# A couple's split moved to the end of its own step, and its inverse twiddle product moved behind the output product

## The chip, the cores and the metric

One NeuronCore of one Trainium2 chip runs the whole kernel. The metric is the device time of one execution in microseconds; the time before is the median of three runs. The profile and the trace are of one more execution.

## The reference, cut to what matters

```
X  = rfft(x, axis=1)                    # x: 4 x 3008 x 256
Yr = Xr @ w_r - Xi @ w_i + b_r
Yi = Xr @ w_i + Xi @ w_r + b_i
Yr, Yi = sign(Y) * max(|Y| - 0.01, 0)   # each part by itself
y  = irfft(Yr + 1j * Yi, n=3008)
h  = y @ w_in                           # 12032 x 256 times 256 x 2048
out = (max(h, 0) + alpha * min(h, 0)) @ w_out
```

## The kernel before

**Numbers.** Every product is made from float32 operands that are split into a rounded part `hi` and a rest `lo`; a product is then three matmuls, hi*hi, hi*lo and lo*hi. A split is a copy on ACT (ScalarE) that makes `hi`, followed by a subtraction on DVE (VectorE) or POOL (GpSimd) that makes `lo`.

**The transforms.** The 3008 points are 94 x 32. A forward transform has a product over 94 points (`forward1`), a trip through DRAM, and a product with twiddle factors (`forward2`), which gives one *unit* of 128 spectrum rows. There are 24 units for each of the four batch rows. Units are handled two at a time as a *couple*: `mix_couple` multiplies both with the mixing weights, `bias_couple` adds the bias, `above_couple` and `shrink_couple` threshold, `split_couple` (ACT, L734) and `rest_couple` (DVE, L963) split the thresholded result `shrunk` into `shr_hi` and `shr_lo`. `inverse2` (PE, L536), once for each unit of the couple, multiplies them with the inverse twiddle factors into PSUM bank 2 of `work_ps`. `copy_couple` (ACT, L739) copies both results to `inv_sb`, and `store_couple` (SP, L330) stores them to DRAM. From there `load_back`, `split_back` and `inverse1` (PE, over 94 points) bring the activations `y`.

**The feed-forward loop.** The main loop has 24 tiles `f` of 502 or 500 tokens, each with 16 steps `m`. In a step PE does `hidden(f, m)` (six matmuls into one of the two banks of `h_ps`), then whatever the transforms have in this step, then `output` of the step two before (LAG = 2; six matmuls into `out_ps`). ACT makes `negpart` of the hidden product (`bend`, L785) and then `g_hi` of the step before (`split_bent`, L794). DVE makes `g_raw` (`bend`, L1008) and then `g_lo` of the step before (`rest_bent`, through the helper at L911). `hidden` waits until the bank it writes has been read by DVE's `bend` two steps earlier; `output(q)` waits for `g_lo` of its step, which DVE makes in its step q + 1, behind `bend(q + 1)`.

**Order.** Each engine works through a list of its own, written out by hand, and stops at a wait until the semaphore is there. For a batch row 1, 2 or 3 the units are spread over a period of 96 steps. Unit j of 24 stands at step 22 + (9 * j // 4) of the period, and odd j closes a couple. With T for that step, the couple's work stands, through `p_couple(f, m, after)` (L78), at these steps before the change:

| step | work of the couple |
| --- | --- |
| T + 2 | `mix_couple` (PE), `bias_couple` (DVE) |
| T + 3 | `above_couple` (ACT), `shrink_couple` (DVE), `split_couple` (ACT, last of the step) |
| T + 4 | `rest_couple` (DVE) |
| T + 5 | `inverse2` twice (PE, ahead of `inverse1` and `output`), `copy_couple` (ACT, in the middle of the step) |
| T + 6 | `store_couple` (SP) |

The next couple's T is 4 or 5 steps later, in turn. Where it is 4, the steps T + 2 and T + 4 hold a unit and T + 3 and T + 5 hold none; where it is 5, the steps T + 3 and T + 5 hold a unit. A unit's step has, on PE, `forward2`; on ACT, `copy_more`, `split_whole`, `split_sum` and for every third unit `split_itw`, a split of the table; on DVE, `whole_spec` and `rest_whole`; on POOL, `sum_spec` and `rest_sum`. Two steps before a unit stand `split_pair` (ACT) and `rest_pair` (DVE). `inverse1` and its splits (`i_unit`, L89) stand at even steps m from 4 on, four to six of them for a tile; `split_back` (ACT) at m = 2, 6 and 10; the transposes of the finished tile (`turn`, DVE) at m = 1.

```
p = p_couple(f, m, 5)
if p is not None:
    inverse2(p - 1)
    inverse2(p)
```

The buffers `shrunk`, `shr_hi`, `shr_lo` and `above` hold one couple. `split_couple` waits for the couple's `shrunk` and for the couple before to have passed `inverse2`. The last third of `mix_couple` writes PSUM bank 2 and waits for `copy_couple` of the couple before.

Of the kernel before, what the change touches and what calls it, by code (L numbers as in the profile page):

```python
# [68 lines left out]
def p_unit(f, m, after):  # L69

    at = f % 6 * STEPS + m - after - 22
    for j in range(PAIRS):
        if f < TILES - 6 and at == 9 * j // 4:
            return PAIRS * (f // 6 + 1) + j
    return None


def p_couple(f, m, after):  # L78

    p = p_unit(f, m, after)  # L80
    return p if p is not None and p % 2 else None
# [19 lines left out]
def mixer_kernel(nc, x, w_r, w_i, b_r, b_i, w_in, w_out, alpha, dft, idft, twiddles, out):  # L101
    with ExitStack() as ctx:  # L102
# [355 lines left out]
        def _(pe):  # L458
# [77 lines left out]
            def inverse2(p):  # L536
                t, k = p // 3 % 2, p % 3
                if k == 0:
                    pe.wait_ge(itw_lo_done, p // 3 + 1)
                pe.wait_ge(shr_lo_done, p + 1)  # L540
                if 2 <= p < PAIRS:
                    pe.wait_ge(inv_copied, p - 1)
                hi, lo = shr_hi[:, p % 2, :], shr_lo[:, p % 2, :]
                product(inv_bank(p), [(itw_hi[:, t, k, :], hi), (itw_hi[:, t, k, :], lo), (itw_lo[:, t, k, :], hi)]
                        ).then_inc(inv_mm, 1)
# [45 lines left out]
            def output(f, m):  # L591
                q = f * STEPS + m
                size = TILE_AT[f % 3][1]
                pe.wait_ge(g_lo_done, q + 1)
                if q == 0:
                    pe.wait_ge(y_lo_done, I_HEAD)
                if f == 0 and m % 2 == 0:
                    pe.wait_ge(wout_lo_done, m // 2 + 1)
                gh, gl = g_hi[:, q % 3, 0:size], g_lo[:, q % 3, 0:size]
                for h in range(DH):  # L600
                    if m == 0 and f >= 1:
                        pe.wait_ge(turned_done, 2 * f - 1 + h)
                    d = slice(h * P, (h + 1) * P)
                    hi, lo = wout_hi[:, m // 2, m % 2, d], wout_lo[:, m // 2, m % 2, d]
                    mm = product(out_ps[:, h, 0:size], [(hi, gh), (hi, gl), (lo, gh)], first=m == 0, last=m == STEPS - 1)
                    if h == 0 and m == STEPS - 1:
                        mm.then_inc(out_half, 1)
                mm.then_inc(out_mm, 1)
# [33 lines left out]
            for f in range(TILES):  # L642
                for m in range(STEPS):
                    hidden(f, m)
                    s = s_unit(f, m)
                    if s is not None:
                        forward1(s)
                    p = p_couple(f, m, 2)
                    if p is not None:
                        mix_couple(p)  # L650
                    p = p_unit(f, m, 0)
                    if p is not None:
                        forward2(p)
                    p = p_couple(f, m, 5)
                    if p is not None:
                        inverse2(p - 1)
                        inverse2(p)
                    u = i_unit(f, m)
                    if u is not None:
                        inverse1(u)  # L660
                    q = f * STEPS + m - LAG
                    if q >= 0:
                        output(*divmod(q, STEPS))
            for m in range(STEPS - LAG, STEPS):
                output(TILES - 1, m)

        @block.scalar
        def _(act):
# [65 lines left out]
            def split_couple(p):  # L734
                act.wait_ge(shrunk_done, p + 1)
                act.wait_ge(inv_mm, p - 1)
                act.activation(shr_hi[:, :, :], shrunk[:, :, :], ACT.Copy).then_inc(shr_hi_done, 2)  # L737

            def copy_couple(p):  # L739
                act.wait_ge(inv_mm, p + 1)  # L740
                if p == PAIRS + 1:
                    for k in range(2):
                        act.wait_ge(inv_stored[k], 16 * GROUPS)
                else:
                    act.wait_ge(couple_stored, 16 * (p - PAIRS - 1) // 2)
                act.activation(inv_sb[:, 0:2, :], work_ps[:, 2, :].rearrange("p (q d) -> p q d", q=2),
                               ACT.Copy).then_inc(inv_copied, 2)
# [25 lines left out]
            def split_y(u):  # L773
                act.wait_ge(back_mm, u + 1)
                if y_free(u) > 0:
                    act.wait_ge(h_mm, STEPS * y_free(u))
                act.activation(y_place(y_hi, u), i_views(u)[0], ACT.Copy).then_inc(y_hi_done, 1)
# [81 lines left out]
            for f in range(TILES):  # L859
                for m in range(STEPS):  # L860
                    bend(f, m)
                    q = f * STEPS + m
                    if q >= 1:
                        split_bent(*divmod(q - 1, STEPS))
                    s = s_unit(f, m)
                    if s is not None:
                        copy_fwd(s)
                    if f == 1 and m in (1, 2):
                        split_mixw(m)
                    p = p_couple(f, m, 3)  # L870
                    if p is not None:
                        above_couple(p)
                    p = p_unit(f, m, 0)
                    if p is not None:
                        copy_more(p)
                    p = p_couple(f, m, 5)
                    if p is not None:
                        copy_couple(p)
                    u = i_unit(f, m)
                    if u is not None:  # L880
                        split_y(u)
                    p = p_unit(f, m, 0)
                    if p is not None:
                        split_whole(p)
                    p = p_unit(f, m, -2)
                    if p is not None:
                        split_pair(p)
                    v = i_bpair(f, m - 2)
                    if v is not None:
                        split_back(v)  # L890
                    if f == 0 and m % 2 == 0 and m // 2 + 2 < CHUNKS:
                        split_ffw(m // 2 + 2)
                    p = p_unit(f, m, -2)
                    if p is not None and p % 3 == 0:
                        split_tw(p // 3)
                    p = p_unit(f, m, 0)
                    if p is not None:
                        split_sum(p)
                        if p % 3 == 0:
                            split_itw(p // 3)  # L900
                    p = p_couple(f, m, 3)
                    if p is not None:
                        split_couple(p)
            split_bent(TILES - 1, STEPS - 1)
            for n in range(1, 12, 2):
                store_out(act, TILES - 1, n)
# [2 lines left out]
        def _(dve):  # L909
# [192 lines left out]
            for f in range(TILES):  # L1102
                for m in range(STEPS):
                    bend(f, m)
                    q = f * STEPS + m
                    if q >= 1:
                        rest_bent(*divmod(q - 1, STEPS))
                    if f >= 1 and m == LAG - 1:
                        turn(f - 1, 0)
                        turn(f - 1, 1)  # L1110
                    if s_unit(f, m + 2) is not None:
                        split_x(s_unit(f, m + 2), False)
                    p = p_couple(f, m, 4)
                    if p is not None:
                        rest_couple(p)
                    p = p_couple(f, m, 3)
                    if p is not None:
                        shrink_couple(p)
                    p = p_couple(f, m, 2)
                    if p is not None:  # L1120
                        bias_couple(p)
                    p = p_unit(f, m, 0)
                    if p is not None:
                        whole_spec(p)
                    u = i_unit(f, m)
                    if u is not None:
                        rest_y(u)
                    p = p_unit(f, m, 0)
                    if p is not None:
                        rest_whole(p)  # L1130
                    if f == 0 and m % 2 == 0 and m // 2 + 2 < CHUNKS:
                        rest_win(m // 2 + 2)
                    p = p_unit(f, m, -2)
                    if p is not None:
                        rest_pair(p)
# [162 lines left out]
```

## Time and profile before

| quantity | value |
| --- | --- |
| median of three runs | 1444.81 us (1444.39 to 1447.1) |
| the profiled execution | 1444.94 us |
| its span, first to last instruction | 1443.1 us |
| mean granted clock of TensorE | 0.991 of full speed |
| busy share: PE, DVE, ACT, POOL | 97%, 65%, 52%, 21% |

The span leaves out 1.8 us of the profiled execution's time, around the first and the last instruction. PE is TensorE; a busy PE is one with a matmul in flight, and since the ends of matmuls are modelled and overlap, a loss of PE time is read from the starts of its matmuls.

### The profile page before, as it was taken

To read this page: it belongs to the slowest core of one execution; us is meant where nothing else is said; L and a number is where in the kernel's file an instruction comes from. 1 tells how busy PE (TensorE), PEld (TensorE's weight loads), DVE (VectorE), ACT (ScalarE), POOL (GpSimd) and SP (SyncE) were. 2 spreads that over 40 slices of the span, in tenths; PEclk is the share of its full clock that TensorE was granted. 3 is DMA by queue.
4 is the path that set the end of the run, shared out by engine and by line. 5 is a ranking of instruction groups with operands and counts; after the bars stand their busy time and mean duration, and the time that the engine had idled before them with its cause. 6 is when DMAs were issued, how large, how long until landed. Compare 5 with 4: busy or idle time off the path is not lost. (4 is left out here: it accounts for less than half of the span.)

```text
span 1443.1 us, 21507 instructions
## 1 busy us (share of the span) xinstructions
PE 1393.5 (97%) x7012; PEld 1171.1 (81%) x7012; DVE 942.3 (65%) x1824; ACT 743.9 (52%) x1646; POOL 301.7 (21%) x351
## 2 busy tenths in 40 slices
PE   8998999999999999998999999999999999999997
PEld 4987888878888888887888888887888888888886
DVE  5786777777765557777775656776776555555554
ACT  3775555555544545655554445565555444444433
POOL 0433532222201422222210241221220110001000
PEclk9999999999999999999999999999999999999999
DMA  6654522122210541213211242222120111001100
GB/s 216 188 153 129 151 66 72 51 63 59 53 38 15 134 107 52 66 47 77 56 33 38 59 114 74 57 67 61 51 55 21 31 26 27 17 19 31 21 15 14
DMA packets 163114, 94.68 MB, mean 66 GB/s; under 512 B 110500, under 2 KB 140628, under 8 KB 163004
## 3 DMA queue, kind: packets, MB, share of 16 engines
q1 hardware_dynamic: 158250, 88.91, 23.4%
q10 hardware_dynamic: 4754, 4.41, 1.0%
q8 instruction: 56, 0.92, 0.3%
q14 instruction: 54, 0.44, 0.1%
HBM read 55.74 MB, written 37.49 MB: 65 GB/s over the span
## 5 line engine op out<-in xcount | busy, mean ns | idle before, releaser
L1008 DVE SCALAR_TENSOR_TENSOR g_raw<-negpart,keep,h_ps 128x502 f32<-128x502 f32 (+1 forms) x384 | 282.8, 736 | 412.9 <-ACT negpart L785 408.0
L785 ACT ACTIVATE negpart<-h_ps 128x502 f32<-128x502 f32 (+1 forms) x384 | 224.7, 585 | 488.8 <-PE h_ps L461 488.8
L461 PE MATMUL out_ps<-g_hi,wout_hi 128*128 128x502 f32 (+1 forms) x768 | 311.9, 406 | 2.8 <-DVE g_lo L911 1.3
L461 PE MATMUL h_ps<-y_hi,win_hi 128*128 128x502 f32 (+1 forms) x768 | 301.2, 392 | 0.6 <-DVE g_raw L1008 0.3
L461 PE MATMUL h_ps<-y_lo,win_hi 128*128 128x502 f32 (+1 forms) x768 | 300.9, 392 | 0.0
L461 PE MATMUL out_ps<-g_hi,wout_lo 128*128 128x502 f32 (+1 forms) x768 | 300.6, 391 | 0.0
L461 PE MATMUL h_ps<-y_hi,win_lo 128*128 128x502 f32 (+1 forms) x768 | 299.9, 390 | 0.0
L461 PE MATMUL out_ps<-g_lo,wout_hi 128*128 128x502 f32 (+1 forms) x768 | 299.8, 390 | 0.0
L911 DVE TENSOR_TENSOR g_lo<-g_raw,g_hi 128x502 fp32r<-128x502 f32 (+1 forms) x384 | 267.9, 698 | 0.1
L794 ACT ACTIVATE g_hi<-g_raw 128x502 fp32r<-128x502 f32 (+1 forms) x384 | 235.9, 614 | 0.3 <-DVE g_raw L1008 0.3
L461 PEld LDWEIGHTS h_ps<-y_hi,win_hi 128*128 128x128 f32 x768 | 146.1, 190 | 32.1 <-DVE y_lo L911 0.8
L461 PEld LDWEIGHTS out_ps<-g_hi,wout_hi 128*128 128x128 f32 x768 | 145.6, 190 | 31.5 <-issue 6.2
L461 PEld LDWEIGHTS h_ps<-y_hi,win_lo 128*128 128x128 f32 x768 | 144.9, 189 | 30.7
L461 PEld LDWEIGHTS out_ps<-g_hi,wout_lo 128*128 128x128 f32 x768 | 145.5, 189 | 30.0
L461 PEld LDWEIGHTS h_ps<-y_lo,win_hi 128*128 128x128 f32 x768 | 145.6, 190 | 29.7
L1143 POOL TENSOR_TENSOR back_lo<-back_raw,back_hi 96x512 fp32r<-96x512 f32 x61 | 83.1, 1362 | 406.1 <-ACT back_hi L771 405.9
L461 PEld LDWEIGHTS out_ps<-g_lo,wout_hi 128*128 128x128 f32 x768 | 146.2, 190 | 22.0
L1165 POOL TENSOR_TENSOR room<-room 128x128 f32<-128x128 f32 x72 | 33.1, 459 | 395.0 <-DVE room L933 395.0
L1143 POOL TENSOR_TENSOR x_lo<-x_raw,x_hi 94x512 fp32r<-94x512 f32 x44 | 56.7, 1289 | 103.7 <-DVE x_hi L917 103.7
L718 ACT ACTIVATE spec_hi<-room 128x256 fp32r<-128x256 f32 x72 | 30.1, 418 | 90.9 <-DVE room L933 90.9
L461 PE MATMUL work_ps<-mixw_lo,spec_hi 128*128 128x256 f32 x216 | 61.0, 282 | 0.0
L461 PE MATMUL work_ps<-mixw_hi,spec_hi 128*128 128x256 f32 x216 | 60.9, 282 | 0.0
(117 smaller groups left out, 1976.4 us busy)
## 6 DMA issues: line engine op xcount, KB each, us to landing
pair_raw<-fwd_scratch SPq DMA_DIRECT2D x96, 128.0 KB, 2.1
back_raw<-inv_scratch SPq DMA_DIRECT2D x61, 192.0 KB, 2.5
table<-in_twiddles_dram SPq DMA_DIRECT2D x28, 384.0 KB, 3.4
x_raw<-in_x_dram SPq DMA_DIRECT2D x64, 160.0 KB
inv_scratch<-inv_sb SPq DMA_DIRECT2D x36, 256.0 KB, 2.2
fwd_scratch<-staging SPq DMA_DIRECT2D x44, 192.0 KB, 2.1
out_dram<-turned SPq DMA_DIRECT2D x124, 40.0 KB, 2.0
inv_scratch<-inv_sb SPq DMA_DIRECT2D x24, 128.0 KB, 2.8
```

Source lines behind the costliest of these rows:

```text
L461: mm = pe.matmul(ps, lhs, rhs, start=(first and n == 0), stop=(last and n == len(terms) - 1), **kw)
L718: act.activation(three(spec_hi)[:, :, 0:2, p % 2, :], spec, ACT.Copy).then_inc(spec_hi_done, 1)
L785: act.activation(negpart[:, q % 2, 0:size], h_ps[:, q % 2, 0:size], ACT.Relu, scale=-1.0).then_inc(negpart_done, 1)
L794: act.activation(g_hi[:, q % 3, 0:size], g_raw[:, q % 2, 0:size], ACT.Copy).then_inc(g_hi_done, 1)
L911: return dve.tensor_tensor(dst, whole, hi.bitcast(F32), ALU.subtract)
L1008: dve.scalar_tensor_tensor(g_raw[:, q % 2, 0:size], negpart[:, q % 2, 0:size], keep[:, m:m + 1], h_ps[:, q % 2, 0:size], ALU.mult, ALU.add ...
L1143: return pool.tensor_tensor(dst, whole, hi.bitcast(F32), ALU.subtract)
L1165: pool.tensor_tensor(spec_sum, spec[:, :, 0, :], spec[:, :, 1, :], ALU.add).then_inc(sum_done, 1)
```

## The change

`rest_couple` moves from DVE's step T + 4, where it stood ahead of `shrink_couple`'s place, to the step T + 3, behind `rest_whole` and ahead of `rest_pair`. `split_couple` moves within ACT's step T + 3 from the last place to the place behind `split_y` and ahead of `split_whole`, `split_pair` and `split_back`. The two `inverse2` stay in step T + 5 and move on PE from the place ahead of `inverse1` to the place behind `output`. `copy_couple` stays in ACT's step T + 5 and moves from the middle of the step to its last place. `store_couple` stays where it is. No instruction is added or taken away, and no wait is changed.

```diff
--- before.py
+++ after.py
@@ -651,16 +651,16 @@
                     p = p_unit(f, m, 0)
                     if p is not None:
                         forward2(p)
-                    p = p_couple(f, m, 5)
-                    if p is not None:
-                        inverse2(p - 1)
-                        inverse2(p)
                     u = i_unit(f, m)
                     if u is not None:
                         inverse1(u)
                     q = f * STEPS + m - LAG
                     if q >= 0:
                         output(*divmod(q, STEPS))
+                    p = p_couple(f, m, 5)
+                    if p is not None:
+                        inverse2(p - 1)
+                        inverse2(p)
             for m in range(STEPS - LAG, STEPS):
                 output(TILES - 1, m)
 
@@ -873,12 +873,12 @@
                     p = p_unit(f, m, 0)
                     if p is not None:
                         copy_more(p)
-                    p = p_couple(f, m, 5)
-                    if p is not None:
-                        copy_couple(p)
                     u = i_unit(f, m)
                     if u is not None:
                         split_y(u)
+                    p = p_couple(f, m, 3)
+                    if p is not None:
+                        split_couple(p)
                     p = p_unit(f, m, 0)
                     if p is not None:
                         split_whole(p)
@@ -898,9 +898,9 @@
                         split_sum(p)
                         if p % 3 == 0:
                             split_itw(p // 3)
-                    p = p_couple(f, m, 3)
-                    if p is not None:
-                        split_couple(p)
+                    p = p_couple(f, m, 5)
+                    if p is not None:
+                        copy_couple(p)
             split_bent(TILES - 1, STEPS - 1)
             for n in range(1, 12, 2):
                 store_out(act, TILES - 1, n)
@@ -1110,9 +1110,6 @@
                         turn(f - 1, 1)
                     if s_unit(f, m + 2) is not None:
                         split_x(s_unit(f, m + 2), False)
-                    p = p_couple(f, m, 4)
-                    if p is not None:
-                        rest_couple(p)
                     p = p_couple(f, m, 3)
                     if p is not None:
                         shrink_couple(p)
@@ -1128,6 +1125,9 @@
                     p = p_unit(f, m, 0)
                     if p is not None:
                         rest_whole(p)
+                    p = p_couple(f, m, 3)
+                    if p is not None:
+                        rest_couple(p)
                     if f == 0 and m % 2 == 0 and m // 2 + 2 < CHUNKS:
                         rest_win(m // 2 + 2)
                     p = p_unit(f, m, -2)
```

## Rows read from the trace of the kernel before

**Rows 1.** The page: busy us of each engine, share of the span, instructions.

```profile
PE 1393.5 (97%) x7012; PEld 1171.1 (81%) x7012; DVE 942.3 (65%) x1824; ACT 743.9 (52%) x1646; POOL 301.7 (21%) x351
```

**Rows 2.** Waits of PE from 200 us on: total us, times, longest us.

```profile
PE work_ps L461 <- DVE shr_lo L911: 25.1, 30, 3.4
```

**Rows 3.** The same view for one period, 205 to 416 us.

```profile
PE work_ps L461 <- DVE shr_lo L911: 8.4, 10, 3.4
```

**Rows 4.** Timeline, first couple: start us, us, engine, operation [idle before <-releaser].

```profile
216.07 0.63 ACT L737 ACTIVATE shr_hi<-shrunk 128x512 fp32r<-128x512 f32 x1 [1.14 <-issue]
...
216.61 0.57 ACT L785 ACTIVATE negpart<-h_ps 128x502 f32<-128x502 f32 x1
...
217.87 0.68 DVE L911 TENSOR_TENSOR g_lo<-g_raw,g_hi 128x502 fp32r<-128x502 f32 x1
...
217.97 0.39 PE L461 MATMUL h_ps<-y_lo,win_hi 128*128 128x502 f32 x1
...
218.21 0.38 PE L461 MATMUL h_ps<-y_hi,win_lo 128*128 128x502 f32 x1
...
218.46 0.68 DVE L911 TENSOR_TENSOR shr_lo<-shrunk,shr_hi 128x512 fp32r<-128x512 f32 x1
...
219.29 0.36 PE L461 MATMUL work_ps<-shr_hi,itw_hi 128*128 128x256 f32 x1 [0.70 <-DVE shr_lo L911]
```

**Rows 5.** Timeline, second couple, whose steps also hold units.

```profile
229.75 0.69 DVE L960 SCALAR_TENSOR_TENSOR shrunk<-biased,above 128x512 f32<-128x512 f32 x1
...
230.81 0.42 ACT L718 ACTIVATE spec_hi<-room 128x256 fp32r<-128x256 f32 x1 [0.94 <-DVE room L933]
...
231.64 0.62 ACT L737 ACTIVATE shr_hi<-shrunk 128x512 fp32r<-128x512 f32 x1
...
233.41 0.67 DVE L911 TENSOR_TENSOR g_lo<-g_raw,g_hi 128x502 fp32r<-128x502 f32 x1
...
233.96 0.22 PE L496 MATMUL work_ps<-tw_parts,pair_lo 128*128 128x128 f32 x1
...
234.74 0.39 PE L461 MATMUL work_ps<-shr_hi,itw_hi 128*128 128x256 f32 x1 [0.56 <-DVE shr_lo L911]
```

**Rows 6.** Timeline, third couple, with an inverse1 product in the same step.

```profile
251.92 0.67 DVE L911 TENSOR_TENSOR g_lo<-g_raw,g_hi 128x500 fp32r<-128x500 f32 x1
...
252.45 0.38 PE L461 MATMUL h_ps<-y_hi,win_lo 128*128 128x500 f32 x1
...
254.06 0.25 PE L567 MATMUL work_ps<-idft_parts,back_hi 96*128 96x188 f32 x1
...
254.44 0.46 PE L461 MATMUL out_ps<-g_hi,wout_hi 128*128 128x500 f32 x1
```

**Rows 7.** Timeline, sixth couple, the longest wait of the period.

```profile
302.43 0.61 ACT L737 ACTIVATE shr_hi<-shrunk 128x512 fp32r<-128x512 f32 x1
...
304.21 0.68 DVE L911 TENSOR_TENSOR g_lo<-g_raw,g_hi 128x502 fp32r<-128x502 f32 x1
...
304.62 1.38 POOL L1143 TENSOR_TENSOR back_lo<-back_raw,back_hi 96x512 fp32r<-96x512 f32 x1 [0.95 <-ACT back_hi L771]
...
304.80 1.76 DVE L911 TENSOR_TENSOR shr_lo<-shrunk,shr_hi 128x512 fp32r<-128x512 f32 x1
...
306.61 0.39 PE L461 MATMUL work_ps<-shr_hi,itw_hi 128*128 128x256 f32 x1 [3.37 <-DVE shr_lo L911]
```

**Rows 8.** Durations of one kind: ns min/median/max, first and last start.

```profile
L911 DVE TENSOR_TENSOR shr_lo<-shrunk,shr_hi x60: 424/682/1759, 43.8 to 1104.2; 128x512 fp32r<-128x512 f32 x36, 128x256 fp32r<-128x256 f32 x24
...
L771 ACT ACTIVATE back_hi<-back_raw x62: 615/622/637, 111.6 to 1362.7; 96x512 fp32r<-96x512 f32 x62
```

**Rows 9.** Busy us by stretches; last three columns: granted clock, DMA share, GB/s.

```profile
307.53:310.94 3.41, 3.41 (x10) 2.72 (x9) 1.36 (x4) 1.41 (x4) 0.99 (x2) 0.50 0.51 150
...
652.28:655.69 3.41, 3.18 (x11) 2.83 (x12) 2.26 (x6) 1.40 (x4) 0.46 (x1) 0.50 0.15 30
...
997.02:1003.85 6.83, 5.50 (x16) 4.73 (x17) 3.61 (x6) 1.92 (x6) 1.71 (x3) 0.50 0.50 136
```

## The prediction, made before the changed kernel ran

> **What bounds the kernel now.** I read four views, in this order. First the page: PE is busy for 97% of the span, DVE for 65% [rows 1]. So only what makes PE stand still, or run slowly, is worth anything. Second, the waits of PE in the main loop, where one line holds nearly all: the inverse twiddle products (on `work_ps`) wait for DVE's `shr_lo`, 25.1 us in 30 waits [rows 2]. Third, the same view for one period of 96 steps: 8.4 us in 10 waits, the longest 3.4 [rows 3]; the other two periods repeat it to the digit. Twelve couples stand in a period, so two of them do not wait. Fourth, the timeline around single waits, to see what is late and why.
>
> A wait's listed idle time is not the whole loss. Matmuls of `hidden` start 0.23 us apart (217.97 to 218.21, with rounding), so after the one at 218.21 the next could start at 218.44; it starts at 219.29. That is 0.85 lost where the row lists 0.70 [rows 4]. With 0.16 more for each wait a period loses 8.4 + 10 x 0.16 = 10.0 us, and the three periods 30.0 us. In period order, the ten losses are 0.85, 0.72, 0.58, 0.80, 3.54 (sixth couple), 0.85, 0.79, 0.57, 0.78 and 0.48 (they are the ten idle times plus 0.16; they add up to the 10.0; rows 4 to 7 show the first, second, third and sixth couple).
>
> In the first couple one sees the mechanism. ACT ends `shr_hi` at 216.70. DVE could subtract then, but its list has `bend` and `rest_bent` of step T + 4 first, so `shr_lo` starts at 218.46 only, behind `g_lo`, and ends at 219.14. PE stands from 218.44 on [rows 4].
>
> Beside the waits there are three stretches in which the granted clock is 0.50, the 1.2 GHz level: 3.41, 3.41 and 6.83 us [rows 9]. Each begins about when a 3.4 us idle stretch of PE ends, that of the sixth couple of a period [rows 7]. They sum to 13.65 us; at half rate they cost at most 6.8 us.
>
> **The change part by part.** Nothing is added: the same instructions run. The sum is only of waits removed and waits that appear.
>
> *rest_couple into T + 3.* One DVE operation, 0.68 us [rows 8], 36 times in the loop. `shr_lo` is then ready about two steps before `inverse2` needs it, so all 30.0 us of the waits for it go. What is late next: `output` of step T + 3, which in T + 5 now comes ahead of `inverse2` and needs `g_lo` of its step. DVE makes that behind `bend` of T + 4, and ahead of that now stands `shr_lo`.
>
> Couples without a unit in T + 3 and T + 5. In the first, `shr_lo` would run from 216.78 to 217.46, overlapping `negpart` (216.61 to 217.18) [rows 4]. `bend` starts at 217.40 where it could start at 217.21, 0.19 later; `g_lo` ends at 218.55 + 0.19 = 218.74; with 0.1 to reach PE, `output` starts at 218.84. PE is there at 218.44, so 0.40 is lost in place of 0.85. The old product started 0.74 behind the end of `g_lo`, the new one 0.29 behind its old end: each such loss shrinks by 0.45. For 0.57 and 0.48 that leaves 0.12 and 0.03. Where `inverse1` is in T + 5, it now runs before `output` and gives the others 0.38 more (254.06 to 254.44 [rows 6]): of 0.58 nothing is left.
>
> Couples with a unit in T + 3. *split_couple ahead of split_whole*: ACT stood idle for 0.94 before `split_whole`, waiting for DVE; `shrunk` is done at 230.44, `split_whole` starts at 230.81, `shr_hi` at 231.64 [rows 5]. `shr_hi` would run from 230.50 to 231.12, `split_whole` 0.23 later than before, and all behind it ends 0.3 earlier. On DVE `rest_whole` waits 0.23 longer, then `shr_lo` and `rest_pair` follow, and `bend` of T + 4 starts about where it did; `g_lo` ends at 234.08 + 0.05. `output` starts at 234.23; PE is there at 234.74 - 0.72 = 234.02. Each such loss shrinks by 0.51: 0.72 to 0.21, 0.80 with an `inverse1` to 0, and 0.78 to between 0 and 0.27; I take 0.2.
>
> Two couples have a `split_back` in T + 3, a copy of 0.62 us [rows 8], that ran while ACT waited for `shrunk` or `rest_whole`, and now runs behind `split_couple`. In the one without a unit (0.85, `inverse1` present) it pushes `negpart` by up to 0.62; the loss is 0.85 - 0.45 - 0.38 + 0.6, less the 0.19 that `shr_lo` no longer pushes: 0.4. In the other (0.79) POOL's subtraction of that load may now start before DVE's `rest_pair`, which is bounded below; I take 0.4 there too.
>
> The sixth couple. `shr_hi` starts at 302.43, behind four other operations of ACT; `g_lo` is done at 304.89; then `shr_lo` takes 1.76 us [rows 7], where the median is 0.68 [rows 8]. It started 0.18 behind a subtraction of POOL that lasts 1.38. In its new place, about 302.2, it starts before POOL's load work and should take 0.7. The chain through ACT shrinks by 0.3, `g_lo` ends at 304.6, `output` starts at 304.7 and PE is there at 306.61 - 3.54 = 303.07: 1.6 lost in place of 3.54.
>
> The couples that did not wait stay at nothing. A period then loses 0.40 + 0.21 + 0 + 0 + 1.6 + 0.4 + 0.4 + 0.12 + 0.2 + 0.03 = 3.4 us in place of 10.0. Three periods save 3 x 6.6 = 19.8 us.
>
> *A meeting with POOL* bounds this from the other side. A DVE subtraction that starts under one of POOL's is longer by up to 1.76 - 0.68 = 1.08 us. If every moved `shr_lo` met one, 36 x 1.08 = 39 us would be added to DVE's list, at most that to PE. If none does, nothing is added. I am near the lower end, since one in twelve does now. On this the Trainium skill ("SBUF — State Buffer", section "Who interferes with whom") says that a DVE instruction with two SBUF inputs and a GpSimd instruction that reads SBUF exclude each other, and that the second to start blocks entirely until the first ends. By that the operation of 304.80 would end 1.20 + 0.68 = 1.88 later; the row has 1.76, so it bears the rule out but for 0.12. It speaks against this change, because every place of `shr_lo` that falls behind a POOL start is charged with POOL's rest; it is rival 3 below.
>
> *inverse2 behind output, copy_couple last.* Six matmuls keep their length. Behind `inverse2` on PE stands only the next `hidden`, which needs nothing from it. `copy_couple` waits at the end of ACT's step T + 5, and behind it stands `negpart` of T + 6, which cannot start before `hidden` of T + 6 ends, 1.4 us after `inverse2`; the copy is shorter. The last third of `mix_couple`, where it comes in T + 6, starts another 1.4 us later. In SP's list `store_couple` may hold `load_pair` and `load_back` by 1 to 2 us; these run several steps ahead. So zero for this part; without that cover it could cost its lateness, up to about 1 us a couple or 36 us, but neither loads nor `inv_sb` show up in PE's waits now. A gain from the order alone is in the 0.38 above.
>
> *The clock.* A PE idle stretch of 1.6 us in place of 3.5 may or may not be followed by the lower level; stretches of 0.9 and less in the loop are not. Between 0 and 6.8 us come back. I take half, 3.4.
>
> Sum: 19.8 + 3.4 = 23.2. The profiled execution took 1444.94 us (span 1443.1 and 1.8 around it), 0.1 above the median of the runs: 1444.9 - 23.2 = 1421.7, so 1422.
>
> **The rivals.** (1) *Everything goes*: the new waits for `g_lo` are hidden too, and the clock never drops. 30.0 + 6.8 gone gives 1408. For it: DVE has 35% to spare. Against it: ACT's chain in the sixth couple is 2 us late by itself. (2) *The wait changes its name*: `shr_lo` delays `g_lo` by its full 0.68, not by 0.19 or 0.05. The new losses are then about 0.5 to 0.6 larger in each of the ten, less where `inverse1` covers: 3.4 + 4.2 = 7.6 a period, saving 3 x 2.4 = 7 us, 1437 to 1438. For it: both stand on the same list. Against: `bend` has to wait for `negpart` anyway, with DVE idle. (3) *Slower, by POOL*: the moved `shr_lo`, or `rest_pair` behind it, starts under a POOL subtraction and stretches to 1.76 in nearly all couples, so that `g_lo` is 1.08 + 0.19 late. A period would lose 3.4 + 12 x 1.08, less 1.5 of slack: 14.9 in place of 10.0, and the time is 1444.9 + 3 x 4.9 = 1460. It decides from 6.6 / 12 = 0.55 us of added lateness per couple; above that the change is slower. Against: POOL is busy for 21% of the span, and DVE's earlier start should mostly come first. (4) *No effect*: ACT makes `shr_hi` so late in either order that `shr_lo` is not earlier: 1444.9. Rows 4 speak against it: `shr_hi` ended 1.76 us before `shr_lo` began.
>
> **How the numbers follow.** Forecast (1415 to 1431) 0.70, rival 1 0.10, rival 2 0.11, rival 3 0.04, rival 4 0.05. The likeliest case gives 1422. The range takes most of the forecast's own and the near parts of rivals 1 and 2: 1411 to 1435. What a measurement of this kernel can tell from no change is 0.2%, 2.9 us. Faster: forecast, rivals 1 and 2, 0.91. Same: rival 4, and a mild form of rival 3, 0.05. Slower: 0.04.
>
> **What would show it.** In the profile after, PE's waits for `shr_lo` in the loop should be near 0 in place of 25.1; waits of `out_ps` for `g_lo` should appear, about 20 of them with 8 to 10 us of loss in total, the longest near 1.5 three times. DVE's `shr_lo` of 512 columns should have 0.68 as its maximum, not 1.76. The stretches at half clock should be fewer or gone. PE's idle time before `inverse2` should be 0. It would be wrong if `g_lo`'s waits total above 20 us (rival 2), if `shr_lo`, `pair_lo` or `g_lo` have a mean well above 0.7 (rival 3), or if a wait of `work_ps` for `inv_sb` or of `negpart` behind `copy_couple` shows that the copy was not free.

## The result, and the profile after

The changed kernel takes 1421.31 us, median of four runs (1420.35 to 1423.1), where the kernel before, run beside it, takes 1445.95 us. The ratio is 0.983, interval 0.9812 to 0.9848: 24.6 us faster. The forecast was 1422, of a range of 1411 to 1435. The profiled execution took 1423.1 us with a span of 1421.3.

The waits of PE from 200 us on, kernel after (total us, times, longest us), answer to [rows 2]:

```profile
PE out_ps L461 <- DVE g_lo L911: 4.2, 10, 0.7
PE work_ps L495 <- DVE pair_lo L911: 2.1, 3, 0.7
PE out_ps L461 <- DVE turned L1057: 0.8, 5, 0.2
```

The 25.1 us for `shr_lo` are gone. Two smaller waits stand in their place: `output` for `g_lo`, which was expected, and `forward2` for `pair_lo`, which was not. One of the ten waits for `g_lo`, of 0.7, stands at the end of the loop, as it did before the change.

The first couple, kernel after, answers to [rows 4]:

```profile
218.21 0.63 ACT L737 ACTIVATE shr_hi<-shrunk 128x512 fp32r<-128x512 f32 x1 [1.15 <-issue]
218.95 0.69 DVE L911 TENSOR_TENSOR shr_lo<-shrunk,shr_hi 128x512 fp32r<-128x512 f32 x1 [0.82 <-ACT shr_hi L737]
219.56 0.73 DVE L1008 SCALAR_TENSOR_TENSOR g_raw<-negpart,keep,h_ps 128x502 f32<-128x502 f32 x1
220.21 0.67 DVE L911 TENSOR_TENSOR g_lo<-g_raw,g_hi 128x502 fp32r<-128x502 f32 x1
220.35 0.38 PE L461 MATMUL h_ps<-y_hi,win_lo 128*128 128x502 f32 x1
220.94 0.49 PE L461 MATMUL out_ps<-g_hi,wout_hi 128*128 128x502 f32 x1 [0.20 <-DVE g_lo L911]
222.40 0.28 PE L461 MATMUL work_ps<-shr_hi,itw_hi 128*128 128x256 f32 x1
```

`shr_lo` now comes before `bend` and `g_lo`. PE could have started at 220.58 and starts `output` at 220.94, when `g_lo` is there: 0.35 lost where 0.85 was, and `inverse2` follows with no wait.

The sixth couple, kernel after, answers to [rows 7]:

```profile
302.28 0.69 DVE L911 TENSOR_TENSOR shr_lo<-shrunk,shr_hi 128x512 fp32r<-128x512 f32 x1
302.49 0.79 POOL L1143 TENSOR_TENSOR spec_lo<-room,spec_hi 128x128 fp32r<-128x128 f32 x1 [0.73 <-ACT spec_hi L722]
302.88 0.68 DVE L911 TENSOR_TENSOR pair_lo<-pair_raw,pair_hi 128x256 fp32r<-128x256 f32 x1
303.24 1.19 POOL L1143 TENSOR_TENSOR itw_lo<-table,itw_hi 128x384 fp32r<-128x384 f32 x1
303.61 0.38 PE L495 MATMUL work_ps<-tw_parts,pair_hi 128*128 128x256 f32 x1 [0.71 <-DVE pair_lo L911]
304.13 0.83 DVE L911 TENSOR_TENSOR g_lo<-g_raw,g_hi 128x502 fp32r<-128x502 f32 x1
305.02 0.50 PE L461 MATMUL out_ps<-g_hi,wout_hi 128*128 128x502 f32 x1 [0.74 <-DVE g_lo L911]
```

Here are two losses, 0.88 at `forward2` (0.71 listed and 0.17 more) and 0.90 at `output`; together 1.78 in place of 3.54. DVE and POOL are seen in turn behind each other: `pair_lo`, now behind `shr_lo`, starts under POOL's operation and takes 0.68, where its median is 0.42.

**The balance.** The losses of one period, from the starts of the matmuls as in the prediction:

| couple | 1 | 2 | 3 | 4 | 5 | 6 | 7 | 8 | 9 | 10 | 11 | 12 | sum |
| --- | --- | --- | --- | --- | --- | --- | --- | --- | --- | --- | --- | --- | --- |
| before | 0.85 | 0.72 | 0.58 | 0.80 | 0 | 3.54 | 0.85 | 0.79 | 0.57 | 0.78 | 0.14 | 0.48 | 10.1 |
| forecast | 0.40 | 0.21 | 0 | 0 | 0 | 1.6 | 0.4 | 0.4 | 0.12 | 0.2 | 0 | 0.03 | 3.4 |
| after | 0.35 | 0.40 | 0 | 0.17 | 0 | 1.78 | 0.27 | 0.30 | 0.16 | 0.13 | 0 | 0 | 3.6 |

(The 0.14 of the eleventh couple has no idle time listed, since it is shorter than the modelled tail of the matmul before; the prediction missed it.) Three periods save 30.3 - 10.7 = 19.6 us. In the loop the three half-clock stretches of [rows 9] are gone, and most of the rest is theirs. The loop, seen from the first and last start of `g_raw` (ns min/median/max, first and last start us; first the kernel before, then after), shows it:

```profile
L1008 DVE SCALAR_TENSOR_TENSOR g_raw<-negpart,keep,h_ps x384: 717/737/743, 124.2 to 1431.9; 128x502 f32<-128x502 f32 x128, 128x500 f32<-128x500 f32 x64
```

```profile
L1008 DVE SCALAR_TENSOR_TENSOR g_raw<-negpart,keep,h_ps x384: 718/737/742, 125.8 to 1410.1; 128x502 f32<-128x502 f32 x128, 128x500 f32<-128x500 f32 x64
```

The loop went from 1307.7 to 1284.3 us, 23.4 less: 19.6 of waits and 3.8 of everything else. The clock alone gave more than 3.8. Two of PE's matmuls in the first half-clock stretch of the kernel before start 0.42 apart, where the same two are 0.23 apart at the full clock:

```profile
308.57 0.62 PE L461 MATMUL out_ps<-g_hi,wout_hi 128*128 128x502 f32 x1
308.99 0.62 PE L461 MATMUL out_ps<-g_lo,wout_hi 128*128 128x502 f32 x1
```

Added up over all starts, the three stretches cost 1.5, 1.5 and 2.6 us, 5.6 in all. Two smaller things go the other way in the kernel after: about 1.1 us in delays of under 0.11 each, most of them at the second matmul behind a wait, which no row of the table counts, and 0.6 us in the loop's first 27 steps, where the clock was still at 0.50 until 127.16. 19.6 + 5.6 - 1.1 - 0.6 is the 23.4 but for 0.1. Ahead of the loop 1.6 us were lost in this execution, where the clock was at 0.50 for longer (kernel after, then before; the last three columns are granted clock, DMA share and GB/s):

```profile
110.10:127.16 17.06, 16.55 (x57) 13.92 (x56) 5.61 (x12) 5.85 (x13) 0.29 (x1) 0.50 0.33 109
```

```profile
44.70:48.12 3.42, 3.42 (x18) 3.42 (x18) 2.02 (x5) 1.78 (x5) 1.53 (x2) 0.50 0.69 193
116.38:123.21 6.83, 6.58 (x23) 5.50 (x23) 1.50 (x5) 1.20 (x4) 0.00 (x0) 0.50 0.56 182
```

The change touches nothing there. 23.4 - 1.6 is the difference of the spans, 21.8.

### The profile page after: what moved, and what is told of

Its sections match the earlier page's. It is cut to its first block and busy times, and to the rows that moved or that the text cites. A ratio compares the mean times of both kernels' runs of the same rounds, so it can differ in the third digit from the quotient of the medians.

```text
span 1421.3 us, 21507 instructions
## 1 busy us (share of the span) xinstructions
PE 1391.1 (98%) x7012; PEld 1168.1 (82%) x7012; DVE 949.9 (67%) x1824; ACT 744.2 (52%) x1646; POOL 306.7 (22%) x351
## 5 line engine op out<-in xcount | busy, mean ns | idle before, releaser
L911 DVE TENSOR_TENSOR g_lo<-g_raw,g_hi 128x502 fp32r<-128x502 f32 (+1 forms) x384 | 271.0, 706 | 0.1
L461 PE MATMUL work_ps<-mixw_hi,spec_lo 128*128 128x256 f32 x216 | 60.8, 282 | 0.0
```

Of the source, the lines that this page charges most:

```text
L461: mm = pe.matmul(ps, lhs, rhs, start=(first and n == 0), stop=(last and n == len(terms) - 1), **kw)
L911: return dve.tensor_tensor(dst, whole, hi.bitcast(F32), ALU.subtract)
```

## The experiments

Each was run in rounds beside the kernel before. `[D]`, `[A]`, `[P]` and `[C]` name the four moves of the change: `rest_couple` on DVE, `split_couple` on ACT, `inverse2` on PE, `copy_couple` on ACT.

| kernel | moves | median us | ratio to before, interval | loss per period |
| --- | --- | --- | --- | --- |
| the full change | D A P C | 1421.31 | 0.9830 (0.9812 to 0.9848) | 3.6 |
| e1 | D | 1425.83 | 0.9866 (0.9851 to 0.9880) | 4.7 |
| e2 | D A | 1413.76 | 0.9788 (0.9775 to 0.9802) | 1.7 |
| e3 | P C | 1421.69 | 0.9835 (0.9815 to 0.9854) | 2.7 |
| e4 | D A, `rest_pair` first | 1413.35 | 0.9785 (0.9772 to 0.9799) | 1.7 |
| e5 | D A P | 1421.22 | 0.9830 (0.9815 to 0.9845) | 3.6 |
| e6 | A P C | 1417.18 | 0.9797 (0.9782 to 0.9813) | 2.3 |
| e7 | D A P C, `rest_pair` first | 1419.92 | 0.9819 (0.9804 to 0.9833) | 3.2 |
| e8 | A | 1445.88 | 0.9999 (0.9986 to 1.0012) | 9.8 |
| e9 | e4, sixth couple as before | 1425.25 | 0.9855 (0.9837 to 0.9873) | 4.2 |
| e10 | before, sixth couple as e4 | 1433.80 | 0.9911 (0.9895 to 0.9927) | 7.5 |
| e11 | e4, `rest_tw` first | 1411.05 | 0.9749 (0.9733 to 0.9766) | 1.1 |

e9, e10 and e11 ran in other rounds than e1 to e8. There the kernel before took 1446.68 us, beside the others 1444.93 to 1445.95, so a distance of 1 to 2 us between medians of different rounds says little.

### The split without the product's move: e1 and e2

e1 moves `rest_couple` alone. e2 adds `split_couple`:

```diff
+p = p_couple(f, m, 3)      # e2: ACT, ahead of split_whole; e1: left last in the step
+if p is not None:
+    split_couple(p)
+p = p_couple(f, m, 3)      # both: DVE, behind rest_whole
+if p is not None:
+    rest_couple(p)
```

> Only rest_couple moves (DVE, step T + 4 to T + 3); ACT's and PE's lists are those of the kernel before. Theory A (PE's loss came from shr_lo standing behind bend and rest_bent, and each product behind it covers what the next operand is late): the waits for shr_lo vanish, but DVE now stands at shr_hi, which ACT still makes last in T + 3, with rest_pair behind it. The sixth couple keeps about 2.7 us of loss, the four couples with a unit 0.2 to 0.7 each, at forward2 for pair_lo. Loss per period 4.3 us in place of 10.0: 17 us less, and 2 to 6 from the clock, about 1424. Rival B (the order on PE is what brings the gain: a product ahead of inverse2 covers its wait): this edit brings under 6 us, above 1439. Rival C (most of the gain is the clock level that no longer drops): as much as the full change only if the half-clock stretches go.

e1 measured 1425.83, where theory A said about 1424. The waits moved to `forward2`, as theory A had it, and in the sixth couple to `output` as well. Rival B falls: the move on DVE alone brings 19 us, with PE's list untouched. Rival C asked for the half-clock stretches. One of the three is gone and two are left, in the first and the third period, 3.41 us each; they cost 3.1 us by the starts of the matmuls. The first stands behind these two waits of the sixth couple:

```profile
302.18 0.39 PE L495 MATMUL work_ps<-tw_parts,pair_hi 128*128 128x256 f32 x1 [1.71 <-DVE pair_lo L911]
304.14 0.50 PE L461 MATMUL out_ps<-g_hi,wout_hi 128*128 128x502 f32 x1 [0.53 <-DVE g_lo L911]
```

```profile
304.52:307.93 3.41, 3.41 (x10) 2.72 (x9) 2.13 (x5) 0.92 (x3) 0.99 (x2) 0.50 0.82 245
```

The second period has the same two waits and no half-clock stretch.

> rest_couple and split_couple move as in the change; inverse2 and copy_couple stay where the kernel before has them. Theory A: inverse2 finds shr_lo ready and, standing ahead of output, gives g_lo 0.77 us more time. The waits of output for g_lo (0.35, 0.40, 0.90, 0.30, 0.16 in a period of the changed kernel) go but for 0.1; what is left is forward2's wait for pair_lo (0.88, 0.17, 0.13, 0.27). Loss per period 1.3 us in place of 3.6: 6 to 7 us faster than the changed kernel, about 1415. Rival B: slower than the changed kernel by several us, since its PE order is undone. Rival C: equal to the changed kernel, 1421.

e2 measured 1413.76, 7.5 us below the full change (theory A: 6 to 7). In its first couple, `inverse2` keeps PE busy while `g_lo` is made:

```profile
219.80 0.68 DVE L911 TENSOR_TENSOR g_lo<-g_raw,g_hi 128x502 fp32r<-128x502 f32 x1
219.94 0.39 PE L461 MATMUL h_ps<-y_hi,win_lo 128*128 128x502 f32 x1
220.17 0.28 PE L461 MATMUL work_ps<-shr_hi,itw_hi 128*128 128x256 f32 x1
...
220.88 0.39 PE L461 MATMUL out_ps<-g_hi,wout_hi 128*128 128x502 f32 x1
```

Its matmuls follow at 0.23 behind `hidden`, and `output` starts at 220.88 without a wait: the 0.35 of the changed kernel is 0. The product's move is what costs (e5 below shows that the copy's is free). Of the 7.5 us the table's losses give 3 x 1.9 = 5.7; the other 1.8 are fewer of the small delays at the second matmul behind a wait. Two losses of size are left in a period: 0.88 in the sixth couple, and 0.53 in the tenth, where `forward2` waits for POOL's `tw_parts` (1.1 us in 3 waits), which the expectation did not name.

### The product's move without the split's: e3, e6, e8

e3 leaves the split alone and moves `inverse2` and `copy_couple`. e6 adds `split_couple`. e8 moves `split_couple` alone. All three keep

```diff
 p = p_couple(f, m, 4)      # DVE, ahead of shrink_couple
 if p is not None:
     rest_couple(p)
```

> Only inverse2 moves behind output and copy_couple to the end of ACT's step; the split of the couple (split_couple, rest_couple) stays as before. Theory A: g_lo is made ahead of shr_lo as before, output starts when g_lo is there, and the output product (1.4 us) covers shr_lo. The losses per period are 0.2 for the first couple, 0.15 for the second, 1.9 to 2.2 for the sixth, 0 to 0.1 for the rest: 2.6 us, about as good as the full change: 1418 to 1421. If the wait only changed its name, the output product would now lose what inverse2 lost, and the time would stay above 1435. Rival B: all of the gain is here, 1421 or less, and e1 and e2 bring little. Rival C: the sixth couple's idle stretch is about 2 us in place of 3.4; if the clock still drops there, 2 to 5 us of the gain are missing.

e3's sixth couple (timeline):

```profile
301.34 0.68 DVE L911 TENSOR_TENSOR g_lo<-g_raw,g_hi 128x502 fp32r<-128x502 f32 x1
...
301.94 1.78 DVE L911 TENSOR_TENSOR shr_lo<-shrunk,shr_hi 128x512 fp32r<-128x512 f32 x1
302.07 0.49 PE L461 MATMUL out_ps<-g_hi,wout_hi 128*128 128x502 f32 x1 [1.69 <-DVE g_lo L911]
...
303.77 0.39 PE L461 MATMUL work_ps<-shr_hi,itw_hi 128*128 128x256 f32 x1
```

`output` covers nearly all of the 1.78 us that `shr_lo` takes. So either move by itself removes most of the loss, and the gains do not add. e3's loss of 2.7 is smaller than the full change's 3.6, yet its median is the same. Its profiled execution took 1416.69 at a mean granted clock of 0.996; the other three took 1420.52 to 1422.99 at 0.992 to 0.988. That is in line with a clock that drops behind the 1.69 us stretch in some executions. In the traced one it dropped behind none of the three; in e1's it did behind two of three waits of 1.7 us. The three slower executions of e3 had no trace, so for them it is not shown.

> The full change less the move of rest_couple: split_couple, inverse2 and copy_couple move, shr_lo is still made in T + 4 behind g_lo. Theory A: output waits for g_lo alone. Per period 0.16 for the first couple, 0.4 for the seventh (split_back behind split_couple), 1.6 for the sixth, 0.2 elsewhere: 2.4 us in place of 10.0, so 23 us less than the kernel before without the clock: 1417 if the clock never drops in the loop, 1420 to 1422 if the 1.6 us stretches still let it drop, as the spread of e3_pe_copy (1416.7 to 1423.0, mean granted clock 0.996 to 0.988) suggests. Rival (rest_couple's move is needed once inverse2 is late): above 1424.

e6 measured 1417.18, as if the clock never dropped, and its four runs had 0.994 to 0.996. It is the full change without `rest_couple`'s move, and it is 4 us faster. That is the plainest sign that, once `inverse2` stands behind `output`, making `shr_lo` early only delays `g_lo` and `pair_lo`.

> Only split_couple moves ahead of split_whole. Theory A: shr_lo stays behind bend and rest_bent of T + 4, so the losses stay; in the five couples with a unit ACT's chain is 0.28 shorter and each loses 0.3 less, the seventh couple loses 0.6 more, since split_back now runs ahead of negpart: 9.2 us a period in place of 10.0, 2 to 3 us less: 1442 to 1443. Rival (ACT's order is the cause of the late shr_lo): 1435 or less.

e8 measured no difference, where theory A said 1442 to 1443. The sixth couple lost 3.13, the second 0.44 and the seventh 1.45, as expected in place and sign, but the other couples with a unit gained 0.1 at most and not 0.3 (measured 0.71, 0.79 and 0.70 at the fourth, eighth and tenth). The rival fell, and theory A's sum for this kernel was 0.6 us a period too good.

### The side moves: e5, e7

e5 keeps the full change but for `copy_couple`; e7 puts `rest_couple` behind `rest_pair`:

```diff
+p = p_couple(f, m, 5)      # e5: ACT, ahead of i_unit, and not last in the step
+if p is not None:
+    copy_couple(p)
...
 p = p_unit(f, m, -2)       # e7: DVE
 if p is not None:
     rest_pair(p)
+p = p_couple(f, m, 3)      # and not behind rest_whole
+if p is not None:
+    rest_couple(p)
```

> The full change, but copy_couple stays in the middle of ACT's step T + 5, where it now waits for an inverse2 that comes only behind output. Theory A: ACT stands about 1 us at that wait and reaches split_y, split_whole and negpart of T + 6 1 to 1.5 us later; but mix_couple and the next output products give PE more than that, so PE loses 0 to 0.5 us a couple at most: 1421 to 1425, the same as the full change within 2 us if the cover holds. Rival: the move of copy_couple is what makes the late inverse2 affordable; then y_lo, spec_lo or g_lo are late in each of the 36 couples by about 0.5 us or more and the time is 1435 or above.

1421.22: the same waits to the digit (`g_lo` 4.2 us in 10, `pair_lo` 2.1 in 3). Moving the copy was worth nothing and cost nothing; the cover held.

> The full change with rest_couple behind rest_pair in DVE's step. Theory A: forward2 no longer waits for pair_lo (0.88 a period in the sixth couple), but output in the same step waits for g_lo, which is no earlier, so the loss only moves from forward2 to output: the same as the full change, 1420 to 1422. If the meeting of rest_pair with POOL (1.1 us longer in the sixth couple and the eighth) were a loss of its own, it would be 2 to 3 us faster, 1418.

1419.92. In the sixth couple `forward2` no longer waits and `output` does:

```profile
302.80 0.50 PE L461 MATMUL out_ps<-g_hi,wout_hi 128*128 128x502 f32 x1 [1.59 <-DVE g_lo L911]
```

1.76 in one place instead of 0.88 + 0.90, but the eighth couple's 0.30 is gone. So the meeting of `rest_pair` with POOL was a loss of its own there, of 0.9 us over three periods, where the rival had 2 to 3. (Its 1.1 us longer is right for the eighth couple; in the sixth `pair_lo` was 0.26 longer.)

> As e2_dve_act, with rest_couple behind rest_pair in DVE's step T + 3. Theory A: pair_lo is ready before forward2 asks, so those waits (0.88, 0.17, 0.13 and 0.27 a period in the changed kernel) go; in the sixth couple output then waits for g_lo instead, about 1.0 us. Loss per period 1.0 to 1.1 us, 0 to 1 us faster than e2_dve_act: 1414 to 1415. Rival (the lock with POOL): shr_lo, now one operation later, starts under POOL's spec_lo or back_lo and stretches to 1.2 or more in several couples; then g_lo is later and the time is 2 to 5 us above e2_dve_act.

e4, the same swap without the product's move, is within 0.5 us of e2: not told apart. Its loss is 1.7 a period, not 1.0 to 1.1: the waits of 0.17 and 0.53 at `forward2` stayed, since they are for POOL's `tw_parts` and not for `pair_lo`. The rival's stretched `shr_lo` is there, at 0.95 in six of the 36, but cost nothing against e2.

### One couple and the clock: e9, e10

```diff
-if p is not None:
+if p is not None and p % PAIRS != 11:      # e9, the places of e4; e10 has == 11 here
...
-if p is not None:
+if p is not None and p % PAIRS == 11:      # e9, the places of before; e10 has != 11 here
```

> e4_pair_first, but the sixth couple of each period (unit 11 of 24) keeps split_couple and rest_couple where the kernel before has them. Only its wait comes back: 3.54 us in place of 0.96, three times, 7.7 us. Theory A: if nothing else hangs on it the time is 1413.35 + 7.7 = 1421.1. Theory C (a share of the gain is the clock, and it hangs on the 3.4 us stretch of idle PE alone): the half-clock stretches of the kernel before come back behind it and cost 1.7 to 2.7 each besides: 1426 to 1429, mean granted clock near 0.990.

> The complement: only the sixth couple's split moves as in e4_pair_first, the other eleven stay as in the kernel before. Their nine losses (6.5 us a period) stay, 3.54 becomes about 1.0: 7.7 us less, 1437.3; with theory C the clock no longer drops in the loop and 5 to 8 us more go: 1429 to 1432. If the clock also answers to the many stretches of 0.4 to 0.7 us, it still drops somewhere and the time is above 1434.

e9 measured 1425.25, 11.9 above e4's median and, by the ratios to the kernel before, 10.1. Of that 7.7 are waits, which leaves 2.4 to 4.2. By the starts of the matmuls in its trace the half-clock stretches cost 4.2 us (2.7 and 1.5). Its stretches at and behind the three waits:

```profile
301.51:308.33 6.83, 5.73 (x17) 4.87 (x18) 3.38 (x6) 1.69 (x6) 1.48 (x3) 0.50 0.53 145
642.84:646.25 3.41, 3.12 (x11) 2.78 (x11) 2.27 (x6) 1.39 (x4) 0.45 (x1) 0.50 0.15 34
978.00:982.70 4.70, 1.33 (x9) 1.05 (x8) 3.55 (x5) 3.73 (x9) 2.87 (x3) 1.00 0.45 123
982.70:990.00 7.30, 7.30 (x41) 6.37 (x42) 4.06 (x9) 3.26 (x9) 0.99 (x2) 1.00 0.51 118
```

At the first two waits the clock went to the 1.2 GHz level, just before their end, for 6.83 and 3.41 us; the third, a 3.4 us idle stretch too (PE is busy for 1.33 of the 4.70 us), was followed by the full 2.4 GHz. e10 measured 1433.80, in place of the 1437.3 that the waits alone would give: 3.5 us of clock. But the 1437.3 starts from 1445, and the kernel before took 1446.68 beside e10; from there 12.9 us are gone, 7.8 of them waits, which leaves 5.1, near the 5.6 that the stretches cost. It has thirty waits with 15.5 us of idle time in the loop, none over 0.7, and no half-clock stretch there. Theory C holds for a share of about 3.5 to 5 us, at the lower end of what it expected, not as the main cause.

### A version that beats both: e11

```diff
+p = p_unit(f, m, -2)       # POOL, ahead of rest_sum, and not behind rest_wout
+if p is not None and p % 3 == 0:
+    rest_tw(p // 3)
```

> e4_pair_first with rest_tw ahead of rest_sum in POOL's step. In e4_pair_first forward2 waits 0.17 and 0.53 us a period for POOL's tw_parts. They should go: 3 x 0.7 = 2.1 us, 1411.3. Rival: the subtraction of tw_parts, 1.0 us long and now earlier, meets shr_lo or pair_lo on DVE and stretches them, so that g_lo is late instead and the time stays at 1413 or rises.

1411.05, 10 us below the full change and 2.3 below e4, in other rounds. PE's waits in its loop:

```profile
PE out_ps L461 <- DVE g_lo L911: 2.0, 4, 0.7
PE out_ps L461 <- DVE turned L1057: 0.8, 5, 0.2
PE work_ps L461 <- DVE shr_lo L911: 0.6, 3, 0.2
```

The listed wait for `tw_parts` is gone and the other three lines are those of e4, to the digit. The rival fell.

## Why the prediction was right, point by point

**The removed wait.** 30.0 us for `shr_lo` were to go, and went: no PE wait for it is left in the loop. In e1 and e3 each half of the change alone takes PE's listed waits for `shr_lo` out of the loop. The prediction treated the two as parts of one effect and did not say that they are two remedies for the same wait.

**The new wait.** Rival 2's mechanism was real, in the small size that the forecast gave it: 0.35 and 0.16 at couples one and nine, for 0.40 and 0.12. The total, 3.6 for 3.4, hides misses of both signs: couples two, four and six lost 0.5 more than forecast, seven, eight and ten 0.3 less. Half of the sixth's 1.78 is at `forward2` for `pair_lo`, a wait that no step of the prediction named. So the sign given for the profile was off too: about 20 waits of `out_ps` for `g_lo` with a loss of 8 to 10 us, the longest near 1.5, where the trace has nine in the couples, 3.5 us listed and 6.4 of loss, the longest 0.74. The step that was off is "`rest_whole` waits 0.23 longer, then `shr_lo` and `rest_pair` follow, and `bend` of T + 4 starts about where it did". The second couple, kernel after, beside [rows 5]:

```profile
233.53 0.69 DVE L911 TENSOR_TENSOR shr_lo<-shrunk,shr_hi 128x512 fp32r<-128x512 f32 x1
233.74 0.80 POOL L1143 TENSOR_TENSOR spec_lo<-room,spec_hi 128x128 fp32r<-128x128 f32 x1 [0.73 <-ACT spec_hi L722]
234.13 0.69 DVE L911 TENSOR_TENSOR pair_lo<-pair_raw,pair_hi 128x256 fp32r<-128x256 f32 x1
234.74 0.72 DVE L1008 SCALAR_TENSOR_TENSOR g_raw<-negpart,keep,h_ps 128x500 f32<-128x500 f32 x1
235.38 0.67 DVE L911 TENSOR_TENSOR g_lo<-g_raw,g_hi 128x502 fp32r<-128x502 f32 x1
236.11 0.49 PE L461 MATMUL out_ps<-g_hi,wout_hi 128*128 128x502 f32 x1 [0.24 <-DVE g_lo L911]
```

`shr_lo` makes POOL late, POOL makes `pair_lo` late (0.69, median 0.42), and `bend` starts as soon as it ends. `g_lo` is 0.2 later than forecast, and that is the whole of 0.40 for 0.21.

**Meetings with POOL** (rival 3). The extremes of two subtractions, kernel after (ns min/median/max, first and last start us):

```profile
L911 DVE TENSOR_TENSOR shr_lo<-shrunk,shr_hi x60: 424/686/694, 43.4 to 1081.0; 128x512 fp32r<-128x512 f32 x36, 128x256 fp32r<-128x256 f32 x24
L911 DVE TENSOR_TENSOR pair_lo<-pair_raw,pair_hi x96: 381/419/1518, 35.9 to 1063.1; 128x256 fp32r<-128x256 f32 x96
```

`shr_lo` was never stretched, as said: its maximum fell from 1759 to 694 ns. But `pair_lo`, whose maximum was 885 ns, now reaches 1518. The victim was the operation queued behind the moved one. The average lateness stayed far under the 0.55 us from which the rival would have decided.

**The clock.** 3.4 us were taken, half of 6.8, and no row was given for the half. By the starts of the matmuls the three stretches had cost 5.6 us, and all of it came back, so the term was 2.2 too small. The sum had nothing for the 1.1 us of small delays and the 0.6 us at the loop's start, which happen to cancel most of that. That 1422 is so near 1421.31 is in part luck; that the waits give 19.6 where 19.8 was forecast is the mechanism, with the misses of both signs above.

**The free moves.** `copy_couple` was put at zero, and e5 measures zero. `inverse2` behind `output` was called nearly free, with "a gain from the order alone" in the 0.38 of `inverse1`. That step failed: the order costs. Ahead of `output`, `inverse2` covers up to 0.71 us (220.17 to 220.88 in e2) of `g_lo`'s lateness in every couple; behind it, it covers nothing, because after the split's move it has nothing to wait for. e2 against the full change gives its price, 7.5 us. It did not change the forecast, since the losses were worked out for the new order, but the text named no cost for it.

## What to carry to other kernels

When a product waits for an operand, make the operand earlier or the product later, and measure each alone: done together they can pay twice for one wait, and here the pair was 7.5 us worse than the better half. In an in-order list, an operation whose operands are ready belongs ahead of the one whose operand is late, as its cover. And after moving an operation, look at what is queued behind it, not only at the moved one.

## What the runs showed that was not expected

DVE and POOL hold each other up in both directions. In the changed kernel's sixth couple POOL's `spec_lo` started 0.21 behind `shr_lo` and took 0.79, where its median before the change was 0.46; `pair_lo` then started under it and took 0.68 for 0.42, POOL's `itw_lo` 1.19 for 1.01, and `g_lo` 0.83 for 0.68: one meeting led to the next. The Trainium skill ("SBUF — State Buffer", section "Who interferes with whom") says that DVE and GpSimd take the port pair that they share as an exclusive lock, and that whichever issues first has it for its whole instruction. The chain above agrees but for 0.14 to 0.15 us: each second one's stretch is that much shorter than the rest of the first.

An idle stretch of 3.4 us on PE was followed by 6.83, 3.41 or no us at 1.2 GHz in one execution (e9). One of 1.7 us with one of 0.5 us close behind it was followed by 3.41, no and 3.41 us (e1), one of 1.7 us alone by none in three (e3). So a single trace gives the cost of the clock only roughly.
